# Block-diagonal stationary matrices for a pair of heads in the hops and the solve of a delta-rule attention

## What is computed

```python
k_n = k / (norm(k) + 1e-6)
state = 0                                   # (B, H, 48, 48)
for t in range(768):
    y[t] = q[t] @ state
    v_old = k_n[t] @ state
    state = state + beta[t] * outer(k_n[t], v[t] - v_old)
```

## Time and profile before

| | |
|---|---|
| median of 3 runs | 842.01 us (841.84 to 842.5) |
| the profiled execution, its own time | 837.97 us |
| its span, first to last instruction | 836.2 us |
| PE busy in the span | 779.1 us (93%), 10976 matmul records |
| PE weight loads busy | 549.9 us (66%), 10976 records |
| DVE busy | 511.4 us (61%) |
| ACT busy | 317.7 us (38%) |
| POOL busy | 164.7 us (20%) |
| mean granted TensorE clock | 0.99 |
| the attention on PE | until 267.4 us |

### The profile page before, as it was taken

The page is one execution under the profiler, slowest core; times in us unless marked ns, Lnnn a source line. Parts: engine busy times, 40 slices in busy tenths (PEclk is TensorE's granted clock), DMA queues, the critical chain, the costliest instruction groups (busy, mean ns, idle before and its releaser), DMA issues.

```text
span 836.2 us, 24883 instructions
## 1 busy us (share of the span) xinstructions
PE 779.1 (93%) x10976; PEld 549.9 (66%) x10976; DVE 511.4 (61%) x1238; ACT 317.7 (38%) x635; POOL 164.7 (20%) x201
## 2 busy tenths in 40 slices
PE   4688888888889999999999999999999999999998
PEld 3687888788878556555656566656566666666664
DVE  4987687777856884723562346365546767757422
ACT  3465466556542360402131224242332443524211
POOL 2541224231200101300130010003122323323100
PEclk9899899999999999999999999999999999999999
DMA  9033433332121231010001000000000000000101
GB/s 208 25 89 84 124 93 86 79 80 60 43 78 39 62 114 57 1 57 0 30 29 58 0 29 29 2 0 1 1 1 2 3 28 20 29 11 29 38 23 53
DMA packets 44813, 37.54 MB, mean 45 GB/s; under 512 B 27360, under 2 KB 38818, under 8 KB 44706
## 3 DMA queue, kind: packets, MB, share of 16 engines
q1 hardware_dynamic: 37925, 30.90, 12.9%
q10 hardware_dynamic: 6781, 5.05, 2.5%
HBM read 26.50 MB, written 4.72 MB: 37 GB/s over the span
## 4 chain that ended last, share of the span: by engine, by line
PE 81%; DVE 7%; issue 5%; ACT 4%; DMA 2%; SPq 0%; POOL 0%; DVEq 0%; ACTq 0%
PE bank L305 15%; PE bank L1081 6%; PE bank L1129 6%; PE bank L1083 6%; PE bank L1128 6%; PE bank L1127 6%; PE bank L1082 6%; PE bank L1065 5%; PE bank L1067 5%; PE bank L1066 5%; PE bank L337 3%; ACT Dy L443 2%; PE bank L360 2%; PE bank L1105 1%; PE bank L1106 1%
## 5 line engine op out<-in xcount | busy, mean ns | idle before, releaser
L1246 ACT ACTIVATE hT_hi<-bank 128x384 f16<-128x384 f32 x96 | 46.6, 489 | 162.9 <-PE bank L1067 162.9
L1520 DVE SCALAR_TENSOR_TENSOR hT_lo<-bank,hT_hi 128x384 f16<-128x384 f32 x96 | 53.3, 556 | 73.5 <-ACT hT_hi L1246 72.9
L1065 PE MATMUL bank<-unT,wA 128*128 128x384 f16 x288 | 94.0, 326 | 2.1 <-DVE hT_lo L1520 2.1
L1081 PE MATMUL bank<-wA,hT_hi 128*128 128x384 f16 x288 | 94.0, 326 | 1.3 <-DVE hT_lo L1520 1.3
L1067 PE MATMUL bank<-unT,wA 128*128 128x384 f16 x288 | 93.9, 326 | 0.0
L1066 PE MATMUL bank<-unT,wA 128*128 128x384 f16 x288 | 93.9, 326 | 0.0
L1083 PE MATMUL bank<-wA,hT_lo 128*128 128x384 f16 x288 | 93.9, 326 | 0.0
L1082 PE MATMUL bank<-wA,hT_hi 128*128 128x384 f16 x288 | 93.9, 326 | 0.0
L305 PE MATMUL bank<-Yv,ET 64*64 64x48 f32 x2304 | 74.4, 218 | 4.2 <-ACT Yv L443 2.9
L305 PEld LDWEIGHTS bank<-Yv,ET 64*64 64x64 f32 x2304 | 72.2, 135 | 6.8 <-ACT Yv L443 5.0
L443 ACT ACTIVATE Yv<-bank,rows 128x384 f32<-128x384 f32 x72 | 40.5, 577 | 69.5 <-PE bank L305 69.3
(11 more groups left out here) (212 smaller groups left out, 1657.4 us busy)
## 6 DMA issues: line engine op xcount, KB each, us to landing
Kb<-k_dram SPq DMA_DIRECT2D x24, 192.0 KB, 3.7
Vv<-v_dram SPq DMA_DIRECT2D x12, 384.0 KB, 3.8
z_first<-w_dram SPq DMA_DIRECT2D x8, 576.0 KB, 4.0
z_first<-wt_dram SPq DMA_DIRECT2D x8, 576.0 KB, 3.6
out_dram<-hT_hi SPq DMA_DIRECT2D x24, 192.0 KB, 1.9
KQ<-q_dram SPq DMA_DIRECT2D x44, 96.0 KB, 2.3
X<-Yo ACTq DMA_DIRECT2D x12, 192.0 KB
X<-Yo ACTq DMA_DIRECT2D x10, 189.0 KB
```

The costliest lines, as they stand in the source:

```text
L1065: pe.matmul(out, w1[0][:, k, cols], unT[0][:, k, :], start=(k == 0), stop=False)
L1081: pe.matmul(out, hT[0][:, f, cols], w2[0][:, f, :], start=(f == 0), stop=False)
L1520: dve.scalar_tensor_tensor(hT[1][:, f, :], bank[3 + m % 3][:, 0:TG * P], 0.0, hT[0][:, f, :], ALU.max, ALU.subtract).then_inc(s_hl, 1)
```

## The change

`ET` and `TT` get a second index, the head that the columns belong to: `[P, NG, 2, C]`. The part of head `h`'s rows and head `h`'s columns is filled, the rest is zero from two memsets at the start. A pair of heads is then one block-diagonal matrix of 128 by 128, and `solve` and `hop` issue one matmul for it where they issued two. `corner` still issues two of 64 by 64, now reading `TT[half[h], g, h]`. `mask_e` writes each head's part by itself, and only columns 16 to 63 (the first 16 are zero by the mask): two instructions of 64 partitions by 8 x 48 instead of one of 128 by 512. `placed` writes each diagonal block by itself, four copies of 32 partitions by 512 instead of two of 128 partitions by 512, with no scale. `KQ` lies elsewhere in SBUF and its slots are numbered one further; nothing else is done to it. Semaphore counts follow.

```diff
-        KQ = sb("KQ", [P, RT, 2, 2, HG, C])
...
-        ET = sb("ET", [P, NG, C])
-        TT = sb("TT", [P, NG, C])
+        ET = sb("ET", [P, NG, 2, C])
+        TT = sb("TT", [P, NG, 2, C])
...
+        KQ = sb("KQ", [P, RT, 2, 2, HG, C])
...
             def corner(n, u):
...
-                pe.wait_ge(s_tt, 2 * n + 2)
+                pe.wait_ge(s_tt, 4 * n + 4)
...
-                    mm = pair(out[:, j * C:(j + 1) * C], Ab[:, n % RA, g], TT[:, g], True, True)
+                    for h in range(2):
+                        mm = pe.matmul(out[half[h], j * C:(j + 1) * C], Ab[half[h], n % RA, g], TT[half[h], g, h], start=True,
+                                       stop=True, skip_group_check=True)
...
             def solve(c):
...
-                        mm = pair(chain(a)[:, j * D:(j + 1) * D], TT[:, g], Yv[:, c % 2, g], j == 0, True)
+                        mm = pe.matmul(chain(a)[:, j * D:(j + 1) * D], TT[:, g].rearrange("p x t -> p (x t)"), Yv[:, c % 2, g],
+                                       start=j == 0, stop=True, skip_group_check=True)
...
             def hop(c, k):
...
-                        mm = pair(chain(a)[:, j * D:(j + 1) * D], ET[:, g], Yv[:, c % 2, g], False, True)
+                        mm = pe.matmul(chain(a)[:, j * D:(j + 1) * D], ET[:, g].rearrange("p x t -> p (x t)"), Yv[:, c % 2, g],
+                                       start=False, stop=True, skip_group_check=True)
...
             def placed(n):
...
                     act.wait_ge(s_Y, 8 * (n - 1) + 2)
-                for y in range(2):
-                    copy(TT[:, :, 2 * BLK * y:2 * BLK * (y + 1)], To[:].rearrange("p g x i -> p g (x i)"),
-                         scale=rows[:, 9 + y:10 + y]).then_inc(s_tt, 1)
+                else:
+                    act.wait_ge(s_ze, 2)
+                for h in range(2):
+                    for y in range(2):
+                        at = slice(h * C + 2 * BLK * y, h * C + 2 * BLK * (y + 1))
+                        copy(TT[at, :, h, 2 * BLK * y:2 * BLK * (y + 1)],
+                             To[at].rearrange("p g x i -> p g (x i)")).then_inc(s_tt, 1)
...
             def mask_e(n, u):
...
-                dve.tensor_tensor(ET[:, grp(u)], ring("E", n, u)[:].rearrange("p (g t) -> p g t", g=HG),
-                                  mE[:].unsqueeze(1).broadcast_to([P, HG, C]), ALU.mult).then_inc(s_et, 1)
+                else:
+                    dve.wait_ge(s_ze, 1)
+                for h in range(2):
+                    dve.tensor_tensor(ET[half[h], grp(u), h, BLK:C],
+                                      ring("E", n, u)[half[h]].rearrange("p (g t) -> p g t", g=HG)[:, :, BLK:C],
+                                      mE[half[h], BLK:C].unsqueeze(1).broadcast_to([C, HG, C - BLK]), ALU.mult).then_inc(s_et, 1)
...
+            dve.memset(ET[:].rearrange("p g x t -> p (g x t)"), 0.0).then_inc(s_ze, 1)
+            dve.memset(TT[:].rearrange("p g x t -> p (g x t)"), 0.0).then_inc(s_ze, 1)
```

More of the change, by code:

```diff
@@ L128, in attention @@
         s_cst, s_id = sem("tables_loaded"), sem("identity_loaded")
-        s_zk, s_zs = sem("K_zeros"), sem("S_zeros")
+        s_zk, s_zs, s_ze = sem("K_zeros"), sem("S_zeros"), sem("E_and_TT_zeros")
         s_kd = [sem(f"k_loaded{i}") for i in range(RK)]
@@ L166, in freed @@
             return {"GP": (s_ab, 4 * n + (0, 2, 1, 3).index(u) + 1), "T": (s_kt, 2 * n + u + 1),
-                    "E": (s_et, 2 * n + u + 1), "O": (s_oe, 2 * n + u + 1)}[kind]
+                    "E": (s_et, 4 * n + 2 * u + 2), "O": (s_oe, 2 * n + u + 1)}[kind]
         def grp(a):
@@ L229, in load_q @@
                         for r in range(2):
-                            sp.dma_start(KQ[feat[r], n % RT, 1, h], A["q"][h, :, n, grp(r)]).then_inc(s_qd[n % RT], 16)
+                            sp.dma_start(KQ[feat[r], (n + 1) % RT, 1, h], A["q"][h, :, n, grp(r)]).then_inc(s_qd[n % RT], 16)
             load_k(0)
@@ L336, in gram @@
                     for h, r in TILES:
-                        mm = pe.matmul(out[r][half[h], j * P:(j + 1) * P], KQ[feat[r], n % RT, 0, h, m],
-                                       KQ[feat[r], n % RT, :, h, m], start=True, stop=True, skip_group_check=True)
+                        mm = pe.matmul(out[r][half[h], j * P:(j + 1) * P], KQ[feat[r], (n + 1) % RT, 0, h, m],
+                                       KQ[feat[r], (n + 1) % RT, :, h, m], start=True, stop=True, skip_group_check=True)
                 mm.then_inc(s_gp, 1)
@@ L359, in predicted @@
                     for h, r in TILES:
-                        mm = pe.matmul(chain(r)[half[h], m * D:(m + 1) * D], KQ[feat[r], c % RT, 0, h, m],
+                        mm = pe.matmul(chain(r)[half[h], m * D:(m + 1) * D], KQ[feat[r], (c + 1) % RT, 0, h, m],
                                        Sv[feat[r], c % 2, h * HG + m], start=m == 0, stop=True, skip_group_check=True)
@@ L366, in solve @@
                     return
-                pe.wait_ge(s_tt, 2 * c + 2)
+                pe.wait_ge(s_tt, 4 * c + 4)
                 for a in range(2):
@@ L393, in queried @@
                         for h, r in TILES:
-                            mm = pe.matmul(out[r][half[h], m], KQ[feat[r], c % RT, 1, h, m], Sv[feat[r], c % 2, h * HG + m],
+                            mm = pe.matmul(out[r][half[h], m], KQ[feat[r], (c + 1) % RT, 1, h, m], Sv[feat[r], c % 2, h * HG + m],
                                            start=m == 0, stop=False, skip_group_check=True)
@@ L459, in turned @@
                     act.wait_ge(s_T, 2 * n + i + 1)
-                    copy(KQ[:, n % RT, 0, :, 4 * i:4 * i + 4].rearrange("p h m t -> p h (m t)"),
+                    copy(KQ[:, (n + 1) % RT, 0, :, 4 * i:4 * i + 4].rearrange("p h m t -> p h (m t)"),
                          ring("T", n, i)[:].rearrange("p (h w) -> p h w", h=2)).then_inc(s_kt, 1)
@@ L530, in _ @@
                 for r in range(2):
-                    act.dma_start(KQ[feat[r], 0, 1, h], A["q"][h, :, 0, grp(r)]).then_inc(s_qd[0], 16)
+                    act.dma_start(KQ[feat[r], 1, 1, h], A["q"][h, :, 0, grp(r)]).then_inc(s_qd[0], 16)
             for src, dst in ((A["mP"], mP[:]), (A["mU"], mU[:]), (A["mE"], mE[:])):
@@ L650, in blocks_out @@
                 if n:
-                    dve.wait_ge(s_tt, 2 * n)
+                    dve.wait_ge(s_tt, 4 * n)
                 dve.transpose(To[:].rearrange("p g x i -> p i (g x)"), Ux[:].rearrange("p i x k -> p i (x k)")).then_inc(s_to, 1)
```

2 lines of the change are left out of this document (1 added, 1 removed).

## The result

The changed kernel takes 1005.76 us in the median (1001.02 to 1017.62, 4 runs) where the kernel before takes 841.92 us (837.78 to 842.5, 4 runs). The ratio is 1.195, with a 95% interval of 1.190 to 1.200: slower by a fifth. The direction was forecast; the size was not. 1006 us lies far above the range of 898 to 950, and the place is that of the second rival, the falling clock, which had 8% and a time of about 1100.

What follows compares the result with a forecast made beforehand. PE was taken as bounded by its instructions' arrival, just under 20 us a chunk, and closely by its work, 17.3 us. Terms 85.4 + 7 - 6 + 3 - 2 - 2 = +85 us gave a 927 us median, range 898 to 950.

Steps and rivals of the forecast that it cites:

- the second rival: Rival: in the hops PE streams less and the clock falls to 1.2 GHz; 172 us more, about 1100 us; 8%.
- Part 1: Solve and hops: a full-width record takes 0.112 us, so a call takes 3.58 us for 1.80; +85.4 us.
- part 2: Around 128 by 128 matmuls: changing between 64-row tiles and the full array costs 0.33 us, 23 times; +7 us.
- Part 3: PE's instruction fetch: 256 of 1296 instructions go from each chunk, returning some "issue" idle time; -6 us, ends 0 and -26.
- Part 4: `placed` on ACT: four copies for two, with a later start and possible waits of `corner`; +3 us, between 1 and 9.
- part 5: The rest: masks, memsets and place of `KQ` 0; third hop's waits for ACT -2 us; fewer half-clock stalls -2 us.
- The full-width load that keeps up with two small ones: Rival: in solve and hops a 128-column record takes 0.058 us and instructions were the bound; 817 us; 4%.
- The one in which load and stream add up: Rival: in solve and hops load and stream run one after the other, 0.154 us a record; about 990 us; 3%.

Runs made afterwards that it cites:

- narrow32: The kernel before, with hops 2 and 3 loading 32 columns of each head's `ET` in place of 64, same result: 841.46 us, 1.001 of before.
- wide96: The changed kernel, with solve and hops streaming the 48 columns of `Yv` twice, the second copy to bank columns nothing reads: 903.91 us, 1.070 of before.
- pairs_new_layout: The changed kernel, with solve and hops both back to two 64 by 64 matmuls for a pair: 845.87 us, 1.001 of before.
- solve_only: The changed kernel, with the hops back to two 64 by 64 matmuls for a pair, only the solve 128 by 128: 869.35 us, 1.028 of before.

## Why the prediction was right and wrong

**The bound of the kernel before** was read rightly: near both the instructions' arrival and PE's work, with the first on top. The distance between the stalls and narrow32 show it.

**Part 1 and part 2, the wider loads and the changes of tile size: right.** I took 3.58 us for a call and 0.33 us for a way into the full array and out of it. At the full clock the four calls of a chunk take 3.70, 3.70, 3.61 and 3.60 us with their share of the changes, 14.6 us, against 7.4 before (1.78, 1.78, 2.00 and 1.80): 12 x 7.2 = 87 us, where the two terms stood at 92. The records' pace is confirmed by the loads of a hop:

```profile
142.93 3.65 PEld L387 LDWEIGHTS bank<-Yv,ET 128*128 128x128 f32 x32 [0.17 <-issue]
```

One load takes 0.192 us by itself (the median of L374's in the changed kernel), so 31 steps are 3.46 us, 0.112 each, the number taken from the rows of L1042. The rule of the Trainium skill ("TensorE: Matmul & The Clock Gate", Part 3, "The mechanism"), that a load overlaps a running matmul only where the row groups differ, does not hold here as it stands: wide96 streams 96 columns from the same rows under a load of 0.112 us, and the step stays.

**Part 3, the instructions: the mechanism right, the size wrong.** I gave back 6 us of the 26 idle by issue. The groups of wide96 in the window 36 to 333 us, which has the full clock and the changed kernel's instructions:

```profile
L391 PE MATMUL bank<-Yv,ET 128*128 128x96 f32 x1152 | 135.0, 276 | 0.0
L378 PE MATMUL bank<-Yv,TT 128*128 128x96 f32 x383 | 46.2, 279 | 0.4 <-issue 0.4
L354 PE MATMUL bank<-TT,AP 64*64 64x64 f32 x704 | 24.9, 224 | 3.7 <-issue 3.5
L309 PE MATMUL bank<-Yv,AP 64*64 64x48 f32 x739 | 24.6, 218 | 4.3 <-issue 4.1 <-PE bank L402 0.2
L341 PE MATMUL bank<-KQ 48*64 48x128 f32 x640 | 22.1, 275 | 0.0
L366 PE MATMUL bank<-Sv,KQ 48*64 48x48 f32 x704 | 15.4, 225 | 4.8 <-issue 4.8
```

0.4 + 3.5 + 4.1 + 4.8 = 12.8 us are left, so 13 came back, twice what I took, and they sit where I said, between `queried` and the end of `corner`. What was too large is "with one packet in hand it still runs dry there for some 2 us a chunk": it is about 1.1. A period of 25.3 and 25.9 us in wide96, and 24.94 in the changed kernel's one chunk at the full clock (138.20 to 163.14), stands against 26.8 forecast. With the clock held, the whole came to 904 us, inside the range of 898 to 950 but 23 below the forecast itself.

**Part 4 and part 5, the copies, the masks, the memsets: right.** Together +1 us by pairs_new_layout, with -2 to +4 as its interval, against +3. The four copies are there, 2.56 us for 1.33, the four masks of 0.55 us each, and the memsets lie in DVE's wait (it still waited 2.1 us for the tables). The third hop waits for ACT no longer (0.0 us idle before L391), as said. In order, the copies and the masks:

```profile
158.47 2.56 ACT L447 ACTIVATE TT<-To 32x512 f32<-32x512 f32 x4
```

```profile
L671 DVE TENSOR_TENSOR ET<-bank,mE 64x384 f32<-64x384 f32 x4 | 2.2, 554 | 0.1
```

The last term of part 5, -2 us for the clock, is another matter.

**The clock: the step that made the forecast wrong.** The sum had it at -2 us, and it cost 95. The step stands in the second rival: "the trace saw the half level only behind stalls of 3 us, and none are added". I took the one kind of occasion in the trace of before for the rule, and even credited 2 us for fewer stalls (part 5). Idle time is one way to lose the clock; PE at work the whole time, but with its loads wide and its streams short, is another, and the kernel before did this nowhere. The rival itself named the right quantity, streaming beside the load, and the right place. Its price, 172 us above the main forecast, was too high, since the clock comes back in most chunks between `queried` and the solve: its cost is 95 us. Its 8% were too low. The rows of before that bore on it were there to be weighed: 48 columns, at half of the 0.085 us that 97 take, fill not quite four tenths of the 0.112 us that I myself had put for a record, and nothing in the trace ran like that for 20 us on end, so that the trace could not exclude the fall, only not show it.

**The other rivals.** The full-width load that keeps up with two small ones is out (0.112 us a record, not 0.072 or less). The one in which load and stream add up is out by wide96.

**What stays open.** By which measure the chip judges PE's activity is not settled: 24 columns on two small tiles lose a little of the clock, 12 lose much, 48 at full width lose much, 96 none, and neither of the two ways of counting that I set against each other gives all of these. What a short idle time adds, as in solve_only, is not tested. The rest of wide96 can be placed nearly whole in the two profiles: from the first `corner` to the dense part it takes 302.3 us where the kernel before takes 236.8, with PE busy for 82.7 us more and idle for 17.2 less (13.3 by issue, 2.9 for ACT, 1.0 for DVE). Its calls, 3.74, 3.75, 3.65 and 3.64 us a chunk, are 89 us of added work; some 6 us of that I cannot place row by row. The medians differ by 59 us and not by 65, since the profiled execution of the kernel before is 6.6 us below the median that wide96 is compared with.

## What to carry to other kernels

Before two small products are merged into one block-diagonal product, compare the loads: two tiles side by side load at the same time, one tile of twice the width takes twice as long, and half the instructions repay that only if their arrival is the bound by more than the added load. The count tells whether it is: idle times by issue that lie the same number of instructions apart, whatever the call, are waits for a packet. Then ask how much PE streams beside its loads in the new form, for as long as the stretch lasts: where a wide float32 load hides a short stream, the clock can halve though PE is never idle, and the granted clock in the windows is the row to look at first. If such a form must be used, try a wider stream under the load: here 96 columns for 48 cost 0.04 us a call and bought back 100 us.

## What the runs showed of the hardware

- TensorE's clock went to the lower level while PE had a matmul in flight all of the time (granted 0.50 in 17.40 us with 17.40 us busy), and doubling the streamed columns under the same loads kept it at 1.00. With 0.01 for the zeros off the diagonal it fell as much (0.869 for 0.872 in the mean, filled).
- Once low, the clock stayed low through 40 us of such work, where the kernel before was back within 5 us. One wide call in a chunk was enough to lose it in six chunks of twelve (solve_only).
- It happens on 64 by 64 tiles too: with 12 streamed columns in place of 48 the kernel before got slower by 4% for doing less.
- A float32 weight load costs by its stationary columns and not by its rows: 2.00 us for 32 records of 128 rows by 64 columns, 3.70 for 128 by 128, where a pair of 64 by 64 side by side takes 1.80. Under the 128 columns, 96 streamed columns cost as much as 48 (3.74).
- PE's instructions arrive one packet of the instruction queue at a time, 256 of them, in the attention before one in 3.94 us, and a stretch of small matmuls outruns that: its idle times lie 125 to 128 matmuls apart or a multiple of that, and taking 0.3 us off a call, with as many instructions, changed nothing.
